# Turning k / F of three sequences with the DMA crossbar instead of TensorE

## The chip, the cores and the metric

The kernel runs on one core of one Trainium2 chip. The metric is the device time of one execution in microseconds (us). TensorE does the matrix products, VectorE (DVE in the rows) and ScalarE (ACT) the elementwise work, GpSimd (POOL) a few small jobs, and SyncE (SP) issues every DMA, all on one hardware queue that 16 DMA engines share.

## What is computed

Gated linear attention over 4 sequences of 768 tokens with 8 heads of 48, then a layer norm with an MLP (384 to 1536 to 384) and a residual, then a Fourier mix over both axes with a second norm, MLP and residual:

```python
for t in range(S):
    state = alpha[:, :, t, :, None] * state + np.einsum('bhd,bhe->bhde', k[:, :, t], v[:, :, t])
    y[:, :, t] = np.einsum('bhd,bhde->bhe', q[:, :, t], state)
...
ch = np.maximum(xn @ w_ch1, 0.0) @ w_ch2        # first MLP, x + ch goes on
...
X = np.fft.fft(np.fft.fft(x, axis=1), axis=2)   # u = x + real(X), then norm, MLP, u + ch
```

Everything is float32.

## The kernel before

The attention is computed in chunks of 128 tokens, all four pairs of heads at once. With F the running product of alpha within a chunk, q is multiplied by F (`q_mul`) and k is divided by it (`k_div`, 112 partitions by 4 x 128 columns). Scores are products of `k_div` and `q_mul`; masked, they are multiplied with v. The state's increment is k transposed times v, so it needs `k_div` with tokens on the partitions: `k_divT`, 128 by 4 x 112. In the kernel before, TensorE turns `k_div` with four transposes into a PSUM bank (`transpose_k`, line 1415), and ScalarE copies the bank to `k_divT` (`copy_kT`, line 780).

Chunks are grouped in units. Sequence 0 is units 0, 1 and 2 (two chunks each); sequences 1 to 3 are units 3 to 8 (three chunks each). The first MLP of unit n runs in 12 slots (j = 0 to 11), and the attention of unit n + 1 is woven into the same slots: this is the order of work on each engine, written out by hand. In a slot TensorE does `pe_up(j)` (9 matmuls of 384 columns into a bank h), `pe_down(j - 2)` (9 matmuls into the accumulators), and then the slot's piece of attention. For the three chunks of a unit these are:

- slots 0, 3, 6: transposes and scores (`scores`, line 1430)
- slots 1, 4, 7: increments (line 1442, waits for `kT_copied`) and the masked product with v (line 1499)
- slots 2, 5, 8: the part that comes from the state (`outputs_carried`, line 1512)

ScalarE does the Relu of slot j (`act_relu`, line 168) and then `side_one`: `copy_kT` in slots 0, 3, 6; `copy_y` (line 794) in 2, 5, 8; two range tests of alpha (`check_above`, `check_below`, line 760) in slots 3 and 4. VectorE does the low half of the split hidden layer (line 173), then masks, state updates (lines 1066 to 1075) and the preparation of coming chunks: `prepare_q` (scan forward, scale q) and `prepare_k` (scan backward, scale k, line 1015), at the slots in `q_slots` and `k_slots`. `k_slots` is `{2: 1, 5: 2}`: chunk 1 in slot 2, chunk 2 in slot 5. Chunk 0 of the next unit is prepared in slot 8 (`next_k_slot`; slot 7 for unit 3, slot 10 for unit 4).

SyncE works through one list. For the unit after the one that is being attended, it loads alpha and q once the range tests are done (`load_qka`, lines 507 to 511), then k, then v (line 517), and then stores the rows of the unit whose MLP is ending (line 521). Twice in the first half of the run it also copies rows of x1 in DRAM into reversed order (`turn_top`, line 540, and `turn_bottom`, line 547); these copies are written with an outer dimension of 3:

```python
def in_thirds(rows):
    return rows.rearrange("r (k c) -> k r c", k=TURN_PARTS)
```

`turn_top(0)` is issued before the loads for unit 7, `turn_bottom(0)` before those for unit 8. The hidden banks h are two, the tiles hT three, so a Relu may be late by about one slot before TensorE waits for it.

Of the kernel before, what the change touches and what calls it, by code (L numbers as in the profile page):

```python
# [7 lines left out]
F32 = mybir.dt.float32  # L8
F32R = mybir.dt.float32r
ALU = mybir.AluOpType  # L10
ACT = mybir.ActivationFunctionType

P = 128
# [33 lines left out]
class Unit:  # L47

    def __init__(self, n, b, c0, size, par):  # L50
        self.n, self.b, self.c0, self.size, self.par = n, b, c0, size, par
        self.base = CHUNKS * b + c0
        self.cols = size * P
        self.scores, self.increments, self.outputs = (0, 3, 6), (1, 4, 7), (2, 5, 8)
        self.q_slots, self.k_slots = {3: 2}, {2: 1, 5: 2}
        self.next_slot, self.next_k_slot, self.next_q_slot = 6, 8, 10
        self.rows_slot, self.range_slot = 9, 3
# [7 lines left out]
    def last(self, c):  # L65
        return self.c0 + c == CHUNKS - 1

    def slot(self, c):
# [15 lines left out]
ONE += [Unit(2 * b + half + 1, b, UT * half, UT, half) for b in range(1, B) for half in range(2)]  # L84
ONE[4].q_slots = {1: 1, 3: 2}
ONE[3].next_k_slot, ONE[3].next_q_slot, ONE[3].rows_slot = 10, None, 8
ONE[-1].k_slots = {2: 1, 4: 2}
N1 = len(ONE)
# [154 lines left out]
def pipeline(nc, qT, kT, aT, v, g_cols, w11, w12, w21, w22, tab_seq, tab_dim, out):  # L243
# [17 lines left out]
    with ExitStack() as ctx:  # L261
# [32 lines left out]
        with ExitStack() as one:  # L294
# [9 lines left out]
            q_mul = sb1("q_mul", [R, UT, PAIRS, P])  # L304
            k_divT = sb1("k_divT", [P, PAIRS, R])
            probs = [sb1(f"probs{i}", [P, PAIRS, P]) for i in range(2)]

# [68 lines left out]
        k_ready = sem("k_ready")  # L376
        kT_summed = sem("kT_summed")
        kT_copied = sem("kT_copied")
        sc_summed = sem("sc_summed")
# [104 lines left out]
        def _(sp):  # L484
# [19 lines left out]

            def load_qka(u):
                chunks = slice(u.c0, u.c0 + UT)
                sp.wait_ge(a_bounded, u.base)
                sp.wait_ge(range_checked, u.n)
                sp.dma_start(a_in[:, :, :], aT[u.b, :, chunks, :]).then_inc(a_loaded, 16)
                sp.wait_ge(q_ready, u.base)  # L510
                sp.dma_start(q_in[:, :, :], qT[u.b, :, chunks, :]).then_inc(q_loaded, 16)
                sp.wait_ge(k_ready, u.base)
                sp.dma_start(k_in[:, :, :], kT[u.b, :, chunks, :]).then_inc(k_loaded, 16)

# [46 lines left out]
            for u in ONE[3:-2]:  # L561
                load_qka(u)
                load_v(u)
                store_x1(u.b - 1, u.c0 // UT)
            for half in range(2):
                sp.wait_ge(stored[half], 16 + 16 * 2)
            turn_top(0, turned[0])
            load_qka(ONE[-2])
            load_v(ONE[-2])
            store_x1(B - 2, 0)  # L570
            turn_bottom(0, turned[0])
            load_qka(ONE[-1])
            load_v(ONE[-1])
            store_x1(B - 2, 1)
            split.dma(sp, TABLES[:PIECES])
            sp.wait_ge(s_ready, ONE_CHUNKS)
            sp.wait_ge(k_ready, ONE_CHUNKS)
# [179 lines left out]
        def _(act):  # L757
# [16 lines left out]
            def check_below(u):  # L774
                act.wait_ge(above_checked, u.n + 1)
                beyond(u, 1).then_inc(range_checked, 1)

            def copy_kT(u, c):
                act.wait_ge(kT_summed, u.base + c + 1)
                act.activation(k_divT[:, :, :], bank[BKU][:, 0:PAIRS * R].rearrange("p (h k) -> p h k", h=PAIRS),  # L780
                               ACT.Copy).then_inc(kT_copied, 1)
# [25 lines left out]

            def side_one(u, slot):
                for c in range(u.size):
                    if slot == u.scores[c]:  # L810
                        copy_kT(u, c)
                    if slot == u.outputs[c]:
                        copy_y(u, c)
                if slot == u.range_slot:
                    check_above(u)
                if slot == u.range_slot + 1:
                    check_below(u)
                for k in TRANSPOSES_ONE.get(slot, ()):
                    high_xT(u, k, g_col[:, k:k + 1])

# [57 lines left out]
            def side_zero(j):  # L879
                if 0 < j < len(ONE_W) - 2:  # L880
                    split.high(act, ONE_W[2 + j])
                side_one(ONE[1], j)

            unit_one(ONE[0], side_zero)
            for u in range(1, N1 - 2):
                unit_one(ONE[u], lambda j: side_one(ONE[u + 1], j))

            for j in range(JH):
                m.act_relu(act, ONE[-2], j)  # L890
                side_one(ONE[-1], j)
                if j == 5:
                    act.wait_ge(s_ready, ONE_CHUNKS)
                    act.wait_ge(k_ready, ONE_CHUNKS)
                if j in (5, 6):
                    split.high(act, TABLES[j - 5])
# [55 lines left out]
        def _(dve):  # L952
# [164 lines left out]
            def side_one(u, following, slot):  # L1117
# [9 lines left out]

                if slot > 1 and u.n != 2:
                    prepare()
# [4 lines left out]
                if slot in u.outputs:  # L1134
                    add_odd(u, u.outputs.index(slot))
                if slot <= 1 or u.n == 2:
                    prepare()
# [268 lines left out]
        def _(pe):  # L1406
# [123 lines left out]
            def side_one(u, slot):  # L1530
                for c in range(u.size):
                    if slot == u.scores[c]:
                        transpose_k(u, c)
                        scores(u, c)
# [220 lines left out]
```

## Time and profile before

| | us |
|---|---|
| median of 3 runs | 770.03 (769.61 to 770.52) |
| profiled execution | 769.62 |
| its span in the trace | 768.1 |
| TensorE busy | 758.4 (99%) |
| VectorE busy | 456.4 (59%) |
| ScalarE busy | 216.2 (28%) |
| GpSimd busy | 56.0 (7%) |

The span is what the trace covers; about 1.5 us of the profiled execution lie around it. The first MLPs with the attention fill about the first 390 us, the second MLPs with the Fourier part the rest. In the timelines below a row is one instruction, or neighbours of one line merged; the first column is its start, the second its length. Matmuls overlap in the array, so what one costs is read from the distance between starts, not from its length.

### The profile page before, as it was taken

What the parts mean: (1) busy time and instruction counts of PE and PEld (TensorE: products, weight loads), DVE (VectorE), ACT (ScalarE), POOL (GpSimd) and SP (SyncE); (2) the same over time, 40 slices, a digit from 0 to 9 for tenths busy, and PEclk for the clock granted to TensorE, in tenths of its full rate; (3) what the DMA queues carried; (4) which work ended last, traced back from release to release, by engine and by line L of the source; (5) the groups of instructions that cost most, each with busy time, mean ns of one, the idle gap of its engine ahead of it and who ended that gap; (6) DMA issues with size and microseconds to landing.
All of it is one profiled execution on the core that took longest, in us unless ns stands there. A gap on an engine that the chain in (4) does not pass through costs nothing.

```text
span 768.1 us, 17057 instructions
## 1 busy us (share of the span) xinstructions
PE 758.4 (99%) x7066; PEld 734.9 (96%) x7066; DVE 456.4 (59%) x1056; ACT 216.2 (28%) x430; POOL 56.0 (7%) x112
## 2 busy tenths in 40 slices
PE   8999999999999999999999999999999999999998
PEld 7889899999999999999999999999999999999998
DVE  7888777756676576675686764347443664342422
ACT  3443232322313223124243332112221223111211
POOL 1100000000000000000005000200021000200000
PEclk9999999999999999999999999999999999999999
DMA  9362223141311413423043421020003000000000
GB/s 243 116 169 74 68 83 90 35 129 43 104 38 65 118 63 100 103 84 135 2 133 128 147 66 52 5 99 32 1 32 103 31 0 31 0 1 32 0 32 32
DMA packets 34956, 54.11 MB, mean 70 GB/s; under 512 B 1932, under 2 KB 29828, under 8 KB 34884
## 3 DMA queue, kind: packets, MB, share of 16 engines
q1 hardware_dynamic: 34884, 53.10, 22.9%
q8 instruction: 52, 0.85, 0.5%
q14 instruction: 20, 0.16, 0.1%
HBM read 43.65 MB, written 13.37 MB: 74 GB/s over the span
## 4 chain that ended last, share of the span: by engine, by line
PE 91%; DVE 5%; issue 3%; ACT 1%; POOL 0%; DMA 0%; POOLq 0%; DVEq 0%; ACTq 0%
PE h L99 14%; PE h L101 12%; PE h L100 12%; PE acc L99 12%; PE acc L101 12%; PE acc L100 12%; PE side_bank L1499 2%; PE side_bank L1521 2%; PE side_bank L100 2%; PE side_bank L101 2%; PE side_bank L1430 2%; PE side_bank L1512 2%; PE side_bank L99 2%; PE side_bank L1442 1%; PE side_bank L1415 1%
## 5 line engine op out<-in xcount | busy, mean ns | idle before, releaser
L173 DVE SCALAR_TENSOR_TENSOR hT_low<-h,hT_high 128x384 fp32r<-128x384 f32 (+1 forms) x204 | 108.2, 531 | 173.4 <-ACT hT_high L168 172.9
L99 PE MATMUL h<-xnT_high,w_high 128*128 128x384 f32 (+1 forms) x612 | 208.1, 340 | 0.9 <-DVE w_low L232 0.9
L168 ACT ACTIVATE hT_high<-h 128x384 fp32r<-128x384 f32 (+1 forms) x204 | 96.4, 473 | 377.0 <-PE h L101 376.8
L101 PE MATMUL h<-xnT_high,w_low 128*128 128x384 f32 (+1 forms) x612 | 199.4, 326 | 0.0
L100 PE MATMUL h<-xnT_low,w_high 128*128 128x384 f32 (+1 forms) x612 | 199.2, 325 | 0.0
L99 PE MATMUL acc<-w_high,hT_high 128*128 128x384 f32 x576 | 194.2, 337 | 1.1 <-DVE hT_low L173 1.1
L101 PE MATMUL acc<-w_high,hT_low 128*128 128x384 f32 x576 | 193.0, 335 | 0.0
L100 PE MATMUL acc<-w_low,hT_high 128*128 128x384 f32 x576 | 192.5, 334 | 0.0
L99 PEld LDWEIGHTS h<-xnT_high,w_high 128*128 128x128 f32 x612 | 115.1, 188 | 5.2 <-DVE w_low L232 1.0
L100 PEld LDWEIGHTS h<-xnT_low,w_high 128*128 128x128 f32 x612 | 115.3, 188 | 0.0
L101 PEld LDWEIGHTS h<-xnT_high,w_low 128*128 128x128 f32 x612 | 115.1, 188 | 0.0
L99 PEld LDWEIGHTS acc<-w_high,hT_high 128*128 128x128 f32 x576 | 108.3, 188 | 1.8 <-DVE hT_low L173 1.7
L100 PEld LDWEIGHTS acc<-w_low,hT_high 128*128 128x128 f32 x576 | 108.4, 188 | 0.0
L101 PEld LDWEIGHTS acc<-w_high,hT_low 128*128 128x128 f32 x576 | 108.1, 188 | 0.0
L992 DVE TENSOR_TENSOR_SCAN F_inv<-a_safe,F_end_inv,zeros 112x127 f32<-112x127 f32 x96 | 38.3, 460 | 0.0
L979 DVE TENSOR_TENSOR_SCAN F<-a_safe,zeros 112x128 f32<-112x128 f32 x96 | 32.8, 404 | 0.3
L640 POOL TENSOR_TENSOR var_eps<-mean_var,eps 128x3 f32<-128x3 f32 (+2 forms) x18 | 5.5, 305 | 355.2 <-DVE mean_var L1082 355.2
L760 ACT ACTIVATE xn_one<-a_in,limits 112x1536 bf16<-112x1536 f32 (+1 forms) x18 | 25.7, 1426 | 5.3 <-DMA a_in<-alpha_dram 5.3
L1499 PE MATMUL side_bank<-v_in,probs 64*64 64x48 f32 x704 | 24.7, 218 | 0.0
L1096 DVE TENSOR_TENSOR xnT_low<-side_bank,xnT_high 128x384 fp32r<-128x384 f32 x24 | 12.5, 554 | 19.8 <-ACT xnT_high L799 19.8
L232 DVE TENSOR_TENSOR w_low<-stage,w_high 128x768 fp32r<-128x768 f32 x24 | 22.6, 949 | 2.4 <-ACT w_high L228 2.2
L1499 PEld LDWEIGHTS side_bank<-v_in,probs 64*64 64x64 f32 x704 | 22.8, 135 | 0.0
(142 smaller groups left out, 757.3 us busy)
## 6 DMA issues: line engine op xcount, KB each, us to landing
stage<-w_dram SPq DMA_DIRECT2D x24, 384.0 KB, 3.4
x_scratch<-x_unit SPq DMA_DIRECT2D x8, 576.0 KB, 3.2
a_in<-alpha_dram SPq DMA_DIRECT2D x6, 672.0 KB, 5.3
q_in<-q_dram SPq DMA_DIRECT2D x6, 672.0 KB, 7.4
k_in<-k_dram SPq DMA_DIRECT2D x6, 672.0 KB, 4.8
v_in<-v_dram SPq DMA_DIRECT2D x6, 576.0 KB, 3.7
xb<-x_scratch SPq DMA_DIRECT2D x4, 576.0 KB, 4.1
xb<-x_turned SPq DMA_DIRECT2D x4, 576.0 KB, 6.9
```

What stands on the lines that cost most here:

```text
L99: pe.matmul(out, wh, xh, start=start, stop=False)
L100: pe.matmul(out, wh, xl, start=False, stop=False)
L101: return pe.matmul(out, wl, xh, start=False, stop=stop)
L168: act.activation(self.hT[0][:, j % H_SLOTS, 0:u.cols], self.hps[j % H_BANKS][:, 0:u.cols], ACT.Relu).then_inc(self.h_high, 1)
L173: dve.scalar_tensor_tensor(out=self.hT[1][:, j % H_SLOTS, 0:u.cols], in0=self.hps[j % H_BANKS][:, 0:u.cols], scalar=0.0, in1=self.hT[0][:, ...
L232: dve.tensor_tensor(self.pieces[n][1][1], self.slot(n), self.pieces[n][1][0], ALU.subtract).then_inc(self.low_done, 1)
L760: return act.activation(excess[:, 0:u.size, :], a_in[:, slots_of(u), :], ACT.Relu, bias=limits[:, i:i + 1], scale=(1.0, -1.0)[i], accum_ou ...
L979: op = dve.tensor_tensor_scan(F[:, s, h, :], a_safe[:, s, h * P:(h + 1) * P], zeros[:, :], 1.0, ALU.mult, ALU.add)
L992: op = dve.tensor_tensor_scan(F_inv[:, s, h, P - 2::-1], a_safe[:, s, first + P - 1:first:-1], zeros[:, 0:P - 1], F_end_inv[:, s, h:h + 1] ...
L1430: op = pe.matmul(score_bank(u, two)[sub, h * SUB:(h + 1) * SUB], k_div[HR[two], s, h, sub], q_mul[HR[two], s, h, sub], start=True, stop=True)
L1499: op = pe.matmul(bank[BSC][sub, cols], probs[head % 2][sub, head // 2, 0:SUB], v_in[sub, s, cols], start=head == 0, stop=False)
L1512: op = pe.matmul(to, q_mul[HR[two], s, h, sub], state[HR[two], (u.state_slot(c), MIDDLE)[i], h, :], start=two == 1 and h == 0, stop=h == P ...
```

## The change

For sequences 1 to 3 (18 of 24 chunks) TensorE no longer turns `k_div`. Instead ScalarE copies it into `k_planes`, taking the 32-bit words apart into two planes of 16-bit halves (`split_k`); SyncE issues one DMA transpose of [112 x 1024] 16-bit elements (`turn_k`, 224 KB), which writes `kT_planes` [128 x 8 x 112]; and ScalarE joins the planes to `k_divT` (`copy_kT`, now from SBUF). Each step waits for the one before; there is one buffer of each.

```diff
-        self.q_slots, self.k_slots = {3: 2}, {2: 1, 5: 2}
+        self.q_slots, self.k_slots, self.split_slots = {3: 2}, {1: 1, 4: 2}, {2: 1, 5: 2}
...
+    def turned_by_dma(self):
+        return self.b > 0
...
-ONE[4].q_slots = {1: 1, 3: 2}
+ONE[4].q_slots = {0: 1, 3: 2}
-ONE[-1].k_slots = {2: 1, 4: 2}
+FIRST_TURNED = CHUNKS
...
+            def turn_k(u, c):
+                if not u.turned_by_dma():
+                    return
+                sp.wait_ge(k_split, u.base + c - FIRST_TURNED + 1)
+                sp.wait_ge(kT_copied, u.base + c)
+                sp.dma_start_transpose(kT_planes[:, :, :], k_planes[:, :]).then_inc(kT_turned, 16)
+
+            def load_unit(u):
+
+                attending = ONE[u.n - 1]
+                turn_k(attending, 1)
+                load_qa(u)
+                turn_k(attending, 2)
+                load_k(u)
+                load_v(u)
+                turn_k(u, 0)
...
             turn_top(0, turned[0])
-            load_qka(ONE[-2])
-            load_v(ONE[-2])
+            load_unit(ONE[-2])
             store_x1(B - 2, 0)
             turn_bottom(0, turned[0])
-            load_qka(ONE[-1])
-            load_v(ONE[-1])
+            load_unit(ONE[-1])
             store_x1(B - 2, 1)
             split.dma(sp, TABLES[:PIECES])
+            turn_k(ONE[-1], 1)
+            turn_k(ONE[-1], 2)
...
+            def split_k(u, c):
+
+                act.wait_ge(k_ready, u.base + c + 1)
+                if u.base + c > FIRST_TURNED:
+                    act.wait_ge(kT_turned, 16 * (u.base + c - FIRST_TURNED))
+                act.activation(k_planes[:, :].rearrange("p (two t) -> p two t", two=2),
+                               flat(k_div[:, u.slot(c), :, :]).bitcast(U16).rearrange("p (t two) -> p two t", two=2),
+                               ACT.Copy).then_inc(k_split, 1)
+
             def copy_kT(u, c):
+                if u.turned_by_dma():
+
+                    act.wait_ge(kT_turned, 16 * (u.base + c - FIRST_TURNED + 1))
+                    act.wait_ge(u_summed, u.base + c)
+                    act.activation(flat(k_divT[:, :, :]).bitcast(U16).rearrange("p (k two) -> p two k", two=2),
+                                   kT_planes[:, :, :].rearrange("p (two h) k -> p two (h k)", two=2),
+                                   ACT.Copy).then_inc(kT_copied, 1)
+                    return
...
+                if slot in u.split_slots and u.turned_by_dma():
+                    split_k(u, u.split_slots[slot])
...
+                if slot == u.next_k_slot + 1 and following and following.turned_by_dma():
+                    split_k(following, 0)
...
-                if slot > 1 and u.n != 2:
+                if slot == 3 and u.n != 2:
                     prepare()
...
-                if slot <= 1 or u.n == 2:
+                if slot != 3 or u.n == 2:
                     prepare()
...
-                        transpose_k(u, c)
+                        if not u.turned_by_dma():
+                            transpose_k(u, c)
```

## Rows read from the trace of the kernel before

**Rows 1.** The page: busy us, share of the span and instructions of each engine.
```profile
PE 758.4 (99%) x7066; PEld 734.9 (96%) x7066; DVE 456.4 (59%) x1056; ACT 216.2 (28%) x430; POOL 56.0 (7%) x112
```

**Rows 2.** Timeline of TensorE: slots 5 and 6 of attending unit 5.
```profile
205.62 0.34 PE L101 MATMUL acc<-w_high,hT_low 128*128 128x384 f32 x1
205.89 0.68 PE L1512 MATMUL side_bank<-state,q_mul 48*64 48x48 f32 x32
...
209.56 0.34 PE L101 MATMUL acc<-w_high,hT_low 128*128 128x384 f32 x1
209.74 0.55 PE L1415 MATMUL side_bank<-ident,k_div 112*128 112x112 f32 x4
210.22 0.69 PE L1430 MATMUL side_bank<-q_mul,k_div 48*64 48x64 f32 x32
```

**Rows 3.** Groups by line and shape: busy us, mean ns, idle time before.
```profile
L228 ACT ACTIVATE w_high<-stage 128x768 fp32r<-128x768 f32 x24 | 20.1, 839 | 4.6 <-DMA stage<-w_dram 2.4 <-PE acc L101 2.1
```

**Rows 4.** Timeline of ScalarE, slots 2 to 4 of attending unit 5.
```profile
193.60 0.49 ACT L794 ACTIVATE x_unit<-side_bank 128x384 f32<-128x384 f32 x1 [1.71 <-PE side_bank L1512]
...
197.72 1.57 ACT L760 ACTIVATE xn_one<-a_in,limits 112x1536 bf16<-112x1536 f32 x1
```

**Rows 5.** Timeline of VectorE, slots 1 and 2 of attending unit 5.
```profile
189.97 0.36 DVE L1075 TENSOR_TENSOR state<-state_sum,F 112x192 f32<-112x192 f32 x1
...
192.40 0.17 DVE L986 RECIPROCAL F_end_inv<-F 112x4 f32<-112x4 f32 x1
...
194.38 0.69 DVE L1015 TENSOR_TENSOR k_div<-k_in,F_inv 112x512 f32<-112x512 f32 x1
```

**Rows 6.** DMA issues by tile: size, and median us from issue to landing.
```profile
x_scratch<-x_unit SPq DMA_DIRECT2D x8, 576.0 KB, 3.2
...
v_in<-v_dram SPq DMA_DIRECT2D x6, 192.0 KB, 7.0
...
out_dram<-u_mirror_out SPq DMA_DIRECT2D x3, 192.0 KB, 1.9
```

**Rows 7.** Timeline of TensorE: increments of unit 3, chunks 1 and 2.
```profile
109.42 0.57 PE L1442 MATMUL side_bank<-v_in,k_divT 64*48 64x48 f32 x32
...
119.44 0.57 PE L1442 MATMUL side_bank<-v_in,k_divT 64*48 64x48 f32 x32
```

**Rows 8.** Timeline of ScalarE: slot 2 of attending unit 3.
```profile
103.91 0.49 ACT L794 ACTIVATE x_unit<-side_bank 128x384 f32<-128x384 f32 x1 [1.31 <-PE side_bank L1512]
```

**Rows 9.** Timeline of the DMA issues (SPq); the length is how long the issue took.
```profile
201.79 0.32 SPq L509 DMA_DIRECT2D a_in<-alpha_dram  x1
...
237.91 5.79 SPq L540 DMA_DIRECT2D x_turned<-x_scratch  x2
...
285.88 8.71 SPq L547 DMA_DIRECT2D x_turned<-x_scratch  x2
300.70 2.86 SPq L509 DMA_DIRECT2D a_in<-alpha_dram  x1
```

**Rows 10.** Windows: busy us of each engine, granted clock, DMA share, GB/s.
```profile
203.00:208.00 5.00, 5.00 (x58) 4.70 (x57) 2.90 (x8) 0.98 (x2) 0.00 (x0) 1.00 0.92 256
208.00:209.00 1.00, 1.00 (x7) 1.00 (x7) 0.47 (x3) 0.49 (x1) 0.00 (x0) 1.00 0.14 37
```

**Rows 11.** The same view around the two reversing copies.
```profile
250.00:252.00 2.00, 2.00 (x68) 1.73 (x66) 0.94 (x3) 1.18 (x2) 0.37 (x1) 1.00 0.22 65
252.00:254.00 2.00, 2.00 (x15) 1.97 (x12) 0.36 (x1) 0.10 (x1) 0.00 (x0) 1.00 0.91 210
...
300.00:304.00 4.00, 4.00 (x79) 3.91 (x79) 1.20 (x4) 1.12 (x3) 0.37 (x1) 1.00 0.22 65
```

**Rows 12.** Timeline of TensorE: increments of chunk 1 in units 5, 6 and 7.
```profile
201.13 0.57 PE L1442 MATMUL side_bank<-v_in,k_divT 64*48 64x48 f32 x32
...
250.59 0.57 PE L1442 MATMUL side_bank<-v_in,k_divT 64*48 64x48 f32 x32
...
300.04 0.57 PE L1442 MATMUL side_bank<-v_in,k_divT 64*48 64x48 f32 x32
```

More of the change, by code:

```diff
@@ L9 @@
 F32R = mybir.dt.float32r
+U16 = mybir.dt.uint16
 ALU = mybir.AluOpType
@@ L305, in pipeline @@
             k_divT = sb1("k_divT", [P, PAIRS, R])
+            k_planes = sb1("k_planes", [R, 2 * PAIRS * P], U16)
+            kT_planes = sb1("kT_planes", [P, 2 * PAIRS, R], U16)
             probs = [sb1(f"probs{i}", [P, PAIRS, P]) for i in range(2)]
@@ L377, in pipeline @@
         kT_summed = sem("kT_summed")
+        k_split = sem("k_split")
+        kT_turned = sem("kT_turned")
         kT_copied = sem("kT_copied")
@@ L503, in load_again, with load_qa @@
                 sp.dma_start(v_in[:, s, :], v[0, :, g, :]).then_inc(first_v[g], 16)
-            def load_qka(u):
+            def load_qa(u):
                 chunks = slice(u.c0, u.c0 + UT)
@@ L511, in load_qka, with load_k @@
                 sp.dma_start(q_in[:, :, :], qT[u.b, :, chunks, :]).then_inc(q_loaded, 16)
+            def load_k(u):
                 sp.wait_ge(k_ready, u.base)
-                sp.dma_start(k_in[:, :, :], kT[u.b, :, chunks, :]).then_inc(k_loaded, 16)
+                sp.dma_start(k_in[:, :, :], kT[u.b, :, u.c0:u.c0 + UT, :]).then_inc(k_loaded, 16)
+            def turn_k(u, c):
[12 more added lines that the diff above has]
+                turn_k(u, 0)
             def load_v(u):
@@ L561, in _ @@
             for u in ONE[3:-2]:
-                load_qka(u)
-                load_v(u)
+                load_unit(u)
                 store_x1(u.b - 1, u.c0 // UT)
@@ L806, in high_first, with side_one @@
                                scale=g_col[:, k:k + 1]).then_inc(xT_high if i else first_high, 1)
-            def side_one(u, slot):
+            def side_one(u, following, slot):
                 for c in range(u.size):
@@ L881, in side_zero @@
                     split.high(act, ONE_W[2 + j])
-                side_one(ONE[1], j)
+                side_one(ONE[1], ONE[2], j)
             unit_one(ONE[0], side_zero)
             for u in range(1, N1 - 2):
-                unit_one(ONE[u], lambda j: side_one(ONE[u + 1], j))
+                unit_one(ONE[u], lambda j: side_one(ONE[u + 1], ONE[u + 2], j))
             for j in range(JH):
                 m.act_relu(act, ONE[-2], j)
-                side_one(ONE[-1], j)
+                side_one(ONE[-1], None, j)
                 if j == 5:
```

## The prediction

> **What bounds the kernel now.** I read the page first. TensorE is busy for 758.4 of 768.1 us, VectorE 456.4, ScalarE 216.2 [rows 1]. So an instruction taken from TensorE is worth its place in TensorE's stream, and work added elsewhere costs nothing until TensorE waits for it. The rest is therefore a question of deadlines, and I read those from the timelines of each engine (who must be done by when), from the list of DMA issues, and from windows of DMA traffic. The kernel repeats itself: units 5, 6 and 7 run with the same spacing (the increments of their chunk 1 start at 201.13, 250.59 and 300.04 [rows 12]), so one unit serves for all, except where the DMA queue holds something else.
>
> **What TensorE gains.** The four transposes stand between the last product of `pe_down` and the scores: that product starts at 209.56, the scores at 210.22, 0.66 us later. Where no transposes stand between, as before the next kind of attention work (205.62 to 205.89), the distance is 0.27 us [rows 2]. So a chunk gives back 0.66 - 0.27 = 0.39 us, and 18 chunks 7.0 us. If the step from products to scores were as short as that from transposes to scores, it would be 0.48 each, 8.6 us.
>
> **What the new chain costs, chunk 1 of an ordinary unit (unit 5).** VectorE: the state update of slot 1 ends at 189.97 + 0.36 = 190.3, the preparation of k lasts from 192.40 to 195.07, 2.7 us [rows 5]; moved behind the state update it is done at 193.0. It delays the low half of slot 2 by about 1 us, which the two spare hidden banks cover. ScalarE: `copy_y` ends at 194.1 [rows 4], so k is ready in time, and the split follows. No row shows a ScalarE copy of 16-bit halves with a stride; the nearest is 128x768 32-bit elements in 839 ns [rows 3], by length 1.1 us for 1024 and 1.0 us for 896 elements. Bounds: half of that (the elements are half as wide) to twice. I take it as it is, since that row is the nearest in kind. Split done at 195.2, DMA issued at 195.3.
>
> The DMA transpose is the large unknown: 224 KB from SBUF to SBUF. The nearest rows are 192 KB from SBUF to DRAM in 1.9 us, 576 KB from SBUF in 3.2 us, and 192 KB that waited behind others in 7.0 us [rows 6]. I call issue to landing X, bound it by 1.9 and 7.0 and take 3.2, the 576 KB row, because the crossbar handles short rows of 16-bit elements and will not be as fast as a plain copy of its size. About 1 us of it is the start (in the windows, loads issued at 201.79 fill the engines from 203 on [rows 9, 10]), so 2.2 us is what remains once its turn has come. The Trainium skill (DMA: Bandwidth & Descriptors, section Latency and other measured facts) states 261 GB/s for a DMA transpose with a non-contiguous middle dimension. By that the 224 KB would move in 0.9 us, and with the page's fixed 2 us the whole would be an estimated 2.9 us; no row here shows a transpose. The sum would be about 1 us better by it.
>
> With X = 3.2 it lands at 198.5, the joining copy ends at 199.5, and the increments want it at 201.13 - 0.39 = 200.7 [rows 12]. It is hidden, with 1.2 us to spare: X may be 4.4. Chunk 2 has the same distances. Its DMA, however, is queued behind the loads of alpha and q. These are issued after the two range tests, which ScalarE now reaches later, since it stands in `copy_kT` until 199.5: each test takes 1.57 us and its accumulator read [rows 4], so with the Relu between them they end near 203.2 and not 201.7. The loads' traffic lasted until about 208.2, 6.4 us after their issue at 201.79 [rows 9, 10]; now until 209.7. Chunk 2's transpose is issued at 208.3, starts at 209.7 and lands at 211.9; copied by 212.9, wanted at about 213.4. Hidden, barely. Chunk 0 of the next unit has over 7 us. In units 4, 5 and 8 I count no loss.
>
> **Unit 3** runs beside an MLP of two chunks, whose slots are shorter. `copy_y` ends at 103.91 + 0.49 = 104.4 [rows 8]; split 105.5, landing 108.7, copy 109.7; increments wanted at 109.42 - 0.39 = 109.0 [rows 7]: 0.7 us lost. Chunk 2: the range tests end at 113.4, the loads' traffic at about 119.4, the transpose lands at 121.6 and is copied at 122.6, wanted at 119.44 + 0.7 - 0.78 = 119.4 [rows 7]: 3.2 us lost. Together 3.9.
>
> **Units 6 and 7** decide. SyncE has issued the reversing copies at 237.91 (`turn_top`) and 285.88 (`turn_bottom`) [rows 9], on the same queue and ahead of `turn_k`. Their traffic runs at 65 GB/s with a share of 0.22, about three and a half engines of 16, until 252 and until 304 [rows 11]: 12 and 16 us of backlog on a few engines. What is issued behind waits: the alpha load of 300.70 took 2.86 us to issue instead of 0.32 [rows 9], and the traffic stayed at 65 GB/s until 304, the other engines doing nothing for it [rows 11]. In the kernel before nobody was in a hurry: the loads come at 251.26 and 300.70. The new transposes of chunk 1 come at 244.8 and 294.7 (rows of unit 5, 49.5 and 98.9 us later), in the middle of the backlog, and their semaphore is full only when the slowest engine is done. So they land at 252 + 2.2 = 254.2 and 304 + 2.2 = 306.2, are copied at 255.2 and 307.2, and are wanted at 250.59 - 0.39 = 250.2 and 300.04 - 0.39 = 299.65 [rows 12]. TensorE stands for 5.0 and 7.5 us. The later range tests push the next loads, and chunk 2 of both loses an estimated 0.5 us each. Queued behind the waiting ScalarE are the range tests and the Relu of slot 4, which TensorE wants only in slot 6, so they add nothing of their own. The Trainium skill (DMA: Bandwidth & Descriptors, section Queues, rings and completion order) says that on each DMA engine descriptors of one issuing queue are consumed in ring order, and that a copy runs on as many engines as its outermost dimensions allow, here 3. The trace agrees with both (share 0.22, blocked issue).
>
> Moving the load of k behind `turn_k` of chunk 2 and the load of the Fourier rows behind the last `turn_k` delays them by a few us; both have over 10 us until VectorE reads them. The added ScalarE work, 18 x (1.1 + 1.0 - 0.5), about 29 us, lies in an engine that is busy 28% [rows 1].
>
> **The sum.** -7.0 (transposes) + 3.9 (unit 3) + 5.0 + 7.5 (units 6 and 7) + 1.0 = +10.4 us. The span goes from 768.1 to 778.5, the profiled execution from 769.6 to 780.0; its median is 0.4 above that, so 780.4. With X = 1.9 unit 3 loses 1.3, the two backlogs 3.7 and 6.2, chunk 2 nothing: +4.2, 774.2. With X = 4.4: unit 3 loses 6.3, the backlogs 6.2 and 8.7, chunk 2 of units 4 to 7 some 1.5 each: +20, 790.
>
> **Rivals.**
>
> Faster, because the backlog doesn't hold the transposes. If the crossbar copy goes by engines or rings that the reversing copies don't use, the 12.5 + 1.0 us fall away. What is left is -7.0 + 3.9 = -3.1, 766.9; with X = 1.9 it is -5.7, 764.3. For it: the share of 0.22 leaves 12 engines free. Against it: the alpha load did not use them. It decides for faster as soon as units 6 and 7 together lose less than 3 us.
>
> Slower by far, because the transpose is slow (X of 6 or more: short rows, much work to issue). Then each chunk 1 and 2 waits in every unit. At X = 6 units 4, 5 and 8 lose 1.6 on each of six chunks, unit 3 9.5, the backlogs 18, chunk 2 of units 6 and 7 3 each: 43 - 7 = +36, 806. Against it: no plain row of this size needs that long unless it queues.
>
> The same mechanism as forecast, and TensorE's clock falls in the two long stalls. Every row of the trace shows a granted clock of 1.00 [rows 10, 11], but none holds an idle TensorE of 5 us. If after each stall it ran at half speed for as long as it had stood, it would lose half of that again, 2.5 + 3.8 = 6.3 us: 786.7. The Trainium skill (TensorE: Matmul & The Clock Gate, Part 1) states that an idle TensorE falls from 2.4 to 1.2 GHz; no run here shows it yet.
>
> No difference (within 0.2%, 1.5 us, which is about what a measurement can tell): the backlog holds only in part, and losses and gain meet.
>
> **How the numbers follow.** Forecast 0.42, clock falling on top of it 0.15, not held 0.22, slow transpose 0.14, no difference 0.07. The likeliest gives 780.4, with its own range 774 to 790. For 8 in 10 I go down to 765, which takes in most of the faster case, and up to 797. Faster by over 0.2% 0.22, within 0.2% 0.07, slower 0.71.
>
> **What would show it.** In the profile after: no L1415 after the first six chunks, and scores 0.27 us behind the last product; the transpose's time from issue to landing near 3 us in units 4, 5 and 8, and no idle TensorE there; idle TensorE of some 5 and 7.5 us ahead of the increments of chunk 1 of units 6 and 7, released by the ScalarE copy, which was itself released by the DMA; a few us ahead of unit 3's chunk 2. The prediction is wrong if the transposes land in the middle of the reversing copies, or if X is above 4.4.

## The result and the profile after

| | before | after |
|---|---|---|
| median, us | 770.06 (769.61 to 770.52) | 789.21 (788.5 to 790.14) |
| profiled execution / its span, us | 769.6 / 768.1 | 790.14 / 788.6 |
| mean granted clock | 1.0 | 0.985 |

The ratio is 1.0249, 95% interval 1.0232 to 1.0267: slower by 19 us. The forecast was 780.4 with a range of 765 to 797. The sign and the places were right, the size was half of what came.

The page of the changed kernel, to be held against [rows 1]: busy time of the engines, the clock in 40 slices, the chain that ended last by engine, and the groups of the joining copy and of the increments (busy us, mean ns | idle time before them and what ended it).

```profile
PE 760.9 (96%) x6994; PEld 735.8 (93%) x6994; DVE 455.6 (58%) x1056; ACT 244.1 (31%) x448; POOL 56.2 (7%) x112
...
PEclk9999998999999999799999999999999999999999
...
PE 85%; DMA 5%; DVE 3%; issue 3%; ACT 2%; SPq 1%; POOL 0%; POOLq 0%; DVEq 0%; ACTq 0%
...
L818 ACT ACTIVATE k_divT<-kT_planes 128x896 uint16<-128x896 uint16 x18 | 22.0, 1222 | 51.9 <-DMA kT_planes<-k_planes 51.9
...
L1489 PE MATMUL side_bank<-v_in,k_divT 64*48 64x48 f32 (+1 forms) x672 | 14.7, 220 | 19.3 <-ACT k_divT L818 19.1
```

TensorE has 72 matmuls fewer (18 x 4) and is nevertheless busy longer, 760.9 against 758.4 us: it ran slower for a while, as the clock row says (8 and 7 in two slices). It stood idle 19.1 us for the joining copy, which itself stood idle 51.9 us for the DMA. Where, the timeline of TensorE says (start, length, instruction; in brackets the idle time before it and who ended it). These are all the waits on the copy:

```profile
110.45 0.57 PE L1489 MATMUL side_bank<-v_in,k_divT 64*48 64x48 f32 x32 [0.46 <-ACT k_divT L818]
...
123.94 0.90 PE L1489 MATMUL side_bank<-v_in,k_divT 64*48 64x48 f32 x32 [3.79 <-ACT k_divT L818]
...
260.19 0.90 PE L1489 MATMUL side_bank<-v_in,k_divT 64*48 64x48 f32 x32 [5.11 <-ACT k_divT L818]
...
319.76 0.89 PE L1489 MATMUL side_bank<-v_in,k_divT 64*48 64x48 f32 x32 [9.70 <-ACT k_divT L818]
```

They are chunks 1 and 2 of unit 3, chunk 1 of unit 6 and chunk 1 of unit 7. The same 32 matmuls last 0.57 us after the first and about 0.90 after the other three: the clock had fallen. Windows over the work behind those three stalls (window, us, busy us of PE, PEld, DVE, ACT, POOL, granted clock, DMA share, GB/s); the clock is back at 1.00 from 130.50, 263.62 and 325.06 on:

```profile
123.94:130.50 6.56, 6.56 (x79) 6.14 (x79) 1.92 (x5) 0.56 (x2) 0.00 (x0) 0.50 0.00 0
...
260.21:263.62 3.41, 3.41 (x67) 3.32 (x68) 1.50 (x5) 3.37 (x5) 0.00 (x0) 0.50 0.02 5
...
319.76:325.06 5.30, 5.30 (x73) 5.21 (x74) 3.31 (x10) 3.40 (x5) 0.36 (x1) 0.50 0.19 24
```

SyncE's issues there, to be held against [rows 9] (the length is how long the issue took):

```profile
113.81 0.32 SPq L517 DMA_DIRECT2D a_in<-alpha_dram  x1
...
117.39 1.22 SPq L530 DMA_TRANSPOSE kT_planes<-k_planes  x1
...
243.09 5.70 SPq L567 DMA_DIRECT2D x_turned<-x_scratch  x2
249.32 7.00 SPq L530 DMA_TRANSPOSE kT_planes<-k_planes  x1
...
296.20 8.96 SPq L574 DMA_DIRECT2D x_turned<-x_scratch  x2
...
305.26 10.58 SPq L530 DMA_TRANSPOSE kT_planes<-k_planes  x1
```

**Where the 20.5 us of the span went.** Each unit begins with ScalarE's first Relu of slot 0; from one to the next is a unit. Timeline of ScalarE, units 3 to 8:

```profile
98.49 0.38 ACT L172 ACTIVATE hT_high<-h 128x256 fp32r<-128x256 f32 x1 [3.12 <-PE h L105]
...
143.37 0.49 ACT L172 ACTIVATE hT_high<-h 128x384 fp32r<-128x384 f32 x1 [2.22 <-PE h L105]
...
191.73 0.49 ACT L172 ACTIVATE hT_high<-h 128x384 fp32r<-128x384 f32 x1 [3.81 <-PE h L105]
...
240.06 0.49 ACT L172 ACTIVATE hT_high<-h 128x384 fp32r<-128x384 f32 x1 [3.81 <-PE h L105]
...
295.05 0.49 ACT L172 ACTIVATE hT_high<-h 128x384 fp32r<-128x384 f32 x1 [3.82 <-PE h L105]
...
355.49 0.49 ACT L172 ACTIVATE hT_high<-h 128x384 fp32r<-128x384 f32 x1 [3.81 <-PE h L105]
```

In the kernel before the same Relus start at 97.23, 135.97, 185.42, 234.88, 284.33 and 333.80; the last three of them:

```profile
234.88 0.49 ACT L168 ACTIVATE hT_high<-h 128x384 fp32r<-128x384 f32 x1 [3.81 <-PE h L101]
...
284.33 0.49 ACT L168 ACTIVATE hT_high<-h 128x384 fp32r<-128x384 f32 x1 [3.81 <-PE h L101]
...
333.80 0.49 ACT L168 ACTIVATE hT_high<-h 128x384 fp32r<-128x384 f32 x1 [3.81 <-PE h L101]
```

Lengths of the units, in us. A clean unit is one without a wait on the copy; unit 3, which is shorter, is held against 38.74 - 1.13.

| | before | after | difference to a clean unit | of it idle | of it clock |
|---|---|---|---|---|---|
| units 4, 5 (clean) | 49.46 | 48.33 | -1.13 against before | 0 | 0 |
| unit 3 | 38.74 | 44.88 | +7.3 | 4.25 | 3.0 |
| unit 6 | 49.46 | 54.99 | +6.7 | 5.1 | 1.6 |
| unit 7 | 49.47 | 60.44 | +12.1 | 9.7 | 2.4 |

The clock's column is what is left after the idle time, 7.0 us in all. The windows above give it a second way: work at half clock loses half its time, and half of 6.56, 3.41 and 5.30 us is 3.3, 1.7 and 2.6, 7.6 in all. So what a stall costs in clock follows from how long TensorE works at half speed behind it, and not from the stall's own length. The gain of six units, 6 x 1.13 = 6.8, against 26.1 of losses makes 19.3; the first 97 us add 1.26 (this execution ran at a clock of 0.83 from 20 to 30 us, before anything of the change had begun). Together 20.5.

### The profile page after: what moved, and what is told of

It reads as the page before. It is cut to its first block, busy times and chain, and to the rows that moved or that the text cites. A ratio compares the mean times of both kernels' runs of the same rounds, so it can differ in the third digit from the quotient of the medians.

```text
span 788.6 us, 16984 instructions
## 1 busy us (share of the span) xinstructions
PE 760.9 (96%) x6994; PEld 735.8 (93%) x6994; DVE 455.6 (58%) x1056; ACT 244.1 (31%) x448; POOL 56.2 (7%) x112
## 4 chain that ended last, share of the span: by engine, by line
PE 85%; DMA 5%; DVE 3%; issue 3%; ACT 2%; SPq 1%; POOL 0%; POOLq 0%; DVEq 0%; ACTq 0%
PE h L103 13%; PE acc L103 11%; PE h L104 11%; PE h L105 11%; PE acc L105 11%; PE acc L104 11%; DMA kT_planes<-k_planes 3%; PE side_bank L1546 2%; PE side_bank L1568 2%; PE side_bank L104 2%; PE side_bank L105 2%; PE side_bank L103 1%; PE side_bank L1489 1%; PE side_bank L1559 1%; PE side_bank L1477 1%
## 5 line engine op out<-in xcount | busy, mean ns | idle before, releaser
L103 PEld LDWEIGHTS h<-xnT_high,w_high 128*128 128x128 f32 x612 | 116.0, 189 | 5.4 <-DVE w_low L236 1.0
L818 ACT ACTIVATE k_divT<-kT_planes 128x896 uint16<-128x896 uint16 x18 | 22.0, 1222 | 51.9 <-DMA kT_planes<-k_planes 51.9
L1489 PEld LDWEIGHTS side_bank<-v_in,k_divT 64*48 64x48 f32 (+1 forms) x672 | 11.6, 130 | 25.3 <-ACT k_divT L818 20.6
L1489 PE MATMUL side_bank<-v_in,k_divT 64*48 64x48 f32 (+1 forms) x672 | 14.7, 220 | 19.3 <-ACT k_divT L818 19.1
L1546 PE MATMUL side_bank<-v_in,probs 64*64 64x48 f32 x704 | 27.2, 230 | 0.0
```

The costliest lines, as they stand in the source:

```text
L103: pe.matmul(out, wh, xh, start=start, stop=False)
L818: act.activation(flat(k_divT[:, :, :]).bitcast(U16).rearrange("p (k two) -> p two k", two=2), kT_planes[:, :, :].rearrange("p (two h) k -> ...
L1489: return pe.matmul(psum[HR[two], h * D:(h + 1) * D], k_divT[rows, h, HR[two]], v_in[rows, c, head * D:(head + 1) * D], start=True, stop=True)
L1546: op = pe.matmul(bank[BSC][sub, cols], probs[head % 2][sub, head // 2, 0:SUB], v_in[sub, s, cols], start=head == 0, stop=False)
```

## The experiments

All kernels start from the changed kernel. A global chunk is 3 (unit - 1) + chunk: 8 is chunk 2 of unit 3, 16 and 19 are chunk 1 of units 6 and 7, 20 is chunk 2 of unit 7. Where TensorE takes a chunk back, the counts that the semaphores are waited for are made per chunk (`dma_before`, `pe_before`), which the diffs leave out.

**Slots alone.** All 24 chunks turned by TensorE; only the preparation of k and q stays in its new slots.

```diff
+BY_PE = set(range(24))
-        return self.b > 0
+        return self.b > 0 and self.base + c not in BY_PE
```

> The changed kernel with every chunk turned by TensorE again: what is left of the change is that k is prepared in slots 1 and 4, unit 4's q in slot 0, and the order of VectorE's work in a slot. Theory (the moved preparation lies in VectorE's idle time): 770.0 within 1 us. Rival (VectorE's low halves come late and TensorE waits): above 772, with idle time of TensorE released by VectorE in units 3 to 8.

Measured: 770.36 (769.67 to 770.85, 10 runs), ratio 0.9995 (0.9982 to 1.0007). The move to slots 1 and 4 costs nothing.

**The two chunks in the backlog back to TensorE.**

```diff
+BY_PE = set(range(6)) | {16, 19}
```

> The changed kernel, but chunk 1 of units 6 and 7 is turned by TensorE as before; the other 16 chunks stay with the DMA. Theory (their transposes wait behind the reversing copies, nothing else in these units is wrong): the two stalls of 5.1 and 9.7 us go, with them the 1.5 and 2.3 us that TensorE lost at half clock behind them, and two chunks of transposes come back (0.8 us): 789.2 - 18.6 + 0.8 = about 771.4. Chunk 2 of both units may now lose up to 1 us, since its spare time is gone. Rival (the transposes are slow wherever they are hurried): the stalls move to chunk 2 of the same units, and the time stays above 780.

Measured: 771.40 (770.81 to 773.09, 10 runs), ratio 1.0014 (1.0001 to 1.0027), clock 0.996. Two chunks of 18 carry 17.8 of the 19 us. The waits left are 0.47 and 3.87 us in unit 3 and 0.72 in chunk 2 of unit 7.

**Three chunks back.** Unit 3's late chunk as well.

```diff
+BY_PE = set(range(6)) | {8, 16, 19}
```

> As the run with two chunks back on TensorE, and chunk 2 of unit 3 as well (the other 15 chunks stay with the DMA). Theory: unit 3's stall of 3.9 us and the 3.0 us lost at half clock behind it go, one chunk of transposes comes back (0.4): 771.4 - 6.5 = 764.9, faster than the kernel before by 5 us; what is left idle is 0.5 us in unit 3's chunk 1 and 0.7 in unit 7's chunk 2. Rival (the time between was hidden elsewhere, the gain per chunk is less than 0.39 us): not below 768.

Measured: 766.34 (765.62 to 767.96, 4 runs), ratio 0.9951 (0.9934 to 0.9968), clock 0.998. The third chunk gave 5.1 us of the 6.5 expected, more than its stall of 3.87 us. In the kernel with two chunks back TensorE works from 122.85 to 128.08 at a granted clock of 0.50 behind that stall, which is gone here. In this trace the clock was at half from 21.39 to 24.80 instead, ahead of anything that the change touches. With 15 chunks on the DMA the kernel is 3.8 us faster than before; 0.46 and 1.03 us of waits are left.

**A lighter backlog.** The reversing copies in 12 parts and not 3, everything else as in the changed kernel.

```diff
-TURN_PARTS = 3
+TURN_PARTS = 12
```

> The changed kernel, but the reversing copies are written in 12 parts of 128 bytes a row instead of 3 of 512 bytes, so they use 12 engines. If their time goes by bytes for each engine, the backlog shrinks to a quarter (12 and 16 us to 3 and 4), the transposes of units 6 and 7 land about 3 us after issue, and the stalls with their clock cost go: 789.2 - 18.6 = 770.6. If it goes by rows (each engine has the same number), the backlog stays as long and now lies on 12 engines: the time stays at 789 or rises. Either way the landing of both transposes follows the end of the copies' traffic.

Measured: 770.93 (769.47 to 772.25, 10 runs), ratio 1.0006 (0.9996 to 1.0015). The whole loss in units 6 and 7 goes although no transpose was moved. Windows of this kernel during the two reversing copies (window, us, busy us of PE, PEld, DVE, ACT, POOL, granted clock, DMA share, GB/s), and its issues:

```profile
246.00:248.00 2.00, 2.00 (x19) 1.98 (x12) 0.36 (x1) 1.54 (x3) 0.00 (x0) 1.00 1.20 130
...
292.00:294.00 2.00, 2.00 (x13) 1.89 (x11) 1.90 (x5) 0.49 (x1) 0.00 (x0) 1.00 1.22 133
```
```profile
247.62 1.28 SPq L530 DMA_TRANSPOSE kT_planes<-k_planes  x1
...
296.35 3.46 SPq L530 DMA_TRANSPOSE kT_planes<-k_planes  x1
```

**The DMA's own queue.** ScalarE issues the transposes itself, right behind its split, so that they share no queue with the reversing copies.

```diff
-                sp.wait_ge(k_split, u.base + c - FIRST_TURNED + 1)
-                sp.wait_ge(kT_copied, u.base + c)
-                sp.dma_start_transpose(kT_planes[:, :, :], k_planes[:, :]).then_inc(kT_turned, 16)
+                return
...
+                act.wait_ge(k_split, u.base + c - FIRST_TURNED + 1)
+                act.wait_ge(kT_copied, u.base + c)
+                act.dma_start_transpose(kT_planes[:, :, :], k_planes[:, :]).then_inc(kT_turned, 16)
```

> The changed kernel, but ScalarE issues the DMA transposes itself, behind its split, so that they come on its own hardware queue; loads and reversing copies stay on SyncE's. Theory A (what holds them is the order of one queue): they land some 3 us after issue also in units 6 and 7, and chunk 2 of unit 3 no longer waits behind the loads; stalls of 14.8 us and 3.8 us of lost clock go, of unit 3's 7.3 us at least 4: 789.2 - 22.6 = about 766, perhaps 1 or 2 us more for the 1.2 us that each issue holds ScalarE. Theory B (the few DMA engines are busy, whatever the queue): the transposes still land when the reversing copies are over, and the time stays within 3 us of 789.

Measured: 795.36 (791.5 to 803.2, 4 runs), ratio 1.0349 (1.0273 to 1.0425). Neither number came. Timeline of TensorE and ScalarE of this kernel:

```profile
126.04 0.89 PE L1490 MATMUL side_bank<-v_in,k_divT 64*48 64x48 f32 x32 [5.71 <-ACT k_divT L819]
263.05 0.57 PE L1490 MATMUL side_bank<-v_in,k_divT 64*48 64x48 f32 x32 [2.57 <-ACT k_divT L819]
315.55 0.57 PE L1490 MATMUL side_bank<-v_in,k_divT 64*48 64x48 f32 x32 [0.95 <-ACT k_divT L819]
332.44 0.57 PE L1490 MATMUL side_bank<-v_in,k_divT 64*48 64x48 f32 x32 [4.17 <-ACT k_divT L819]
```
```profile
116.69 1.24 ACTq L812 DMA_TRANSPOSE kT_planes<-k_planes  x1
124.79 1.20 ACT L819 ACTIVATE k_divT<-kT_planes 128x896 uint16<-128x896 uint16 x1 [6.38 <-DMA kT_planes<-k_planes]
```

The backlog lost its hold: chunk 1 of unit 6 waits 2.57 and not 5.11 us, that of unit 7 0.95 and not 9.70, and no issue of a transpose takes over 2.2 us. The reversing copies' last packets end at 263.50 and 322.08, the transposes land at 261.78 and 314.27, before them. But chunk 2 came later in every unit, in unit 3 8.1 us after its issue (116.69 to 124.79) against 5.3. What had changed there is that the loads were no longer behind it: SyncE issued the load of k at 115.60, 1.1 us ahead of the transpose, on another queue. That is a suspicion until the load is taken away.

**The loads held back.** As the kernel before this one, but SyncE issues the loads of k and v only after chunk 2's transpose has landed; and in a second kernel those of alpha and q too, for which it also calls `turn_k(attending, 2)` ahead of `load_qa(u)`.

```diff
-                return
+                if u.turned_by_dma() and c == 2:
+                    sp.wait_ge(kT_turned, 16 * (u.base + c - FIRST_TURNED + 1))
```

> ScalarE issues the transposes from its own queue, as in the run before of that kind, but SyncE issues the loads of k and v only after chunk 2's transpose has landed, so that of the loads only alpha and q are in flight beside it. Theory S (the late chunk 2 comes from sharing the 16 engines with the loads): the landing of chunk 2, 5.2 to 8.4 us without the hold, falls to 4 to 6 us, since alpha and q, issued about 3 us ahead of it, are done about 4 us after its issue; unit 3's stall of 5.71 us falls to some 3, unit 7's of 4.17 to some 2, and the kernel from 795 to about 788. Theory Q (a transpose on ScalarE's queue is slow by itself when another queue is active at all, or a landing there is seen late): chunk 2 stays at 5.2 to 8.4, and the time at 795 or above.

> As the kernel with the hold, but SyncE holds back all four loads, alpha and q too, until chunk 2's transpose has landed: nothing else is in flight beside it. Theory S: chunk 2 lands 2.9 to 3.3 us after its issue in every unit, as on an idle machine; unit 3's stall falls to about 1 us (5.71 less 8.1 - 3.0), the stalls of chunk 1 of units 6 and 7 (2.57, 0.95) stay. Against the first theory would be a landing of chunk 2 above 4 us. The time then depends on whether the loads, some 6 us later, are still in time for VectorE: about 780 if they are, with new waits of VectorE on alpha or q if they are not.

Measured: 778.43 (776.31 to 780.55, 4 runs), ratio 1.0098 (1.0079 to 1.0116) with k and v held; 792.95 (789.92 to 796.47), ratio 1.0311 (1.0276 to 1.0345) with all four. The chunk 2 transposes land, from issue to the start of the copy, in units 3 to 8:

| us | 3 | 4 | 5 | 6 | 7 | 8 |
|---|---|---|---|---|---|---|
| own queue | 8.1 | 5.2 | 6.7 | 6.0 | 8.4 | 6.7 |
| k, v held | 5.6 | 4.1 | 4.2 | 3.8 | 3.0 | 2.9 |
| all four held | 4.6 | 3.0 | 3.0 | 3.5 | 3.0 | 2.9 |

So a transpose on ScalarE's queue is not slow by itself, and the chunk 2 transposes were late because they shared the engines with the loads; holding two of them gave 17 us, to 778 where 788 was expected. One landing speaks against that alone: with all four loads held, unit 3's took 4.6 us, and above 4 us had been named as a sign against the theory. No load ran beside it, but one instruction packet of 16 KB did (queue, kind, packets, MB, share of the engines between 116.0 and 121.5):

```profile
q10 hardware_dynamic: 928, 0.23, 22.8%
q8 instruction: 1, 0.02, 1.1%
```

That packet held its engine for 0.94 us, in the middle of the transpose's packets. Over all traces kept here the 88 transposes beside which nothing else ran landed 2.89 to 2.95 us after their issue, and the 29 beside which only instruction packets ran 2.91 to 4.55 us. No kernel here moves these packets, so their part is read from the traces and not tested.

ScalarE of the kernel with k and v held in unit 3, and VectorE of the one with all four held:

```profile
116.61 1.24 ACTq L811 DMA_TRANSPOSE kT_planes<-k_planes  x1
122.24 1.20 ACT L818 ACTIVATE k_divT<-kT_planes 128x896 uint16<-128x896 uint16 x1 [3.91 <-DMA kT_planes<-k_planes]
```
```profile
125.81 0.96 DVE L1017 TENSOR_SCALAR a_safe<-a_in 112x1536 f32<-112x1536 f32 x1 [6.30 <-issue]
```

The second shows where the time of the other went: VectorE stood 6.30 us ahead of its first read of alpha in unit 3 (that load was issued at 121.23 and landed 4.5 us later), 26.7 us in five units, and TensorE waited behind it, 13.1 us in five waits on the state. I had expected about 780 and given the loads of alpha and q room that they do not have. Chunk 1 of units 6 and 7 still landed 7.1 and 7.4 us after its issue with k and v held (7.0 and 5.4 without the hold), and TensorE waited 2.59 and 2.88 us: the own queue weakens the backlog, but does not remove it.

**The clock.** To learn what the halved clock costs, TensorE works instead of standing: 128x128 matmuls of the identity, ahead of the increments of chunks 8, 16 and 19, into a bank that is overwritten; a wait for `u_read` ahead of the scores lets the bank be read first. First 30, 42 and 80 of them, then half.

```diff
+                for _ in range({8: 15, 16: 21, 19: 40}.get(g, 0)):
+                    pe.matmul(bank[BKU][:, 0:P], ident[:, :], ident[:, :], start=True, stop=True)
...
+                        elif u.base + c in {8, 16, 19}:
+                            pe.wait_ge(u_read, u.base + c)
```

> The changed kernel with small matmuls on the identity put into TensorE's stream ahead of the three increments that wait long: 30 in unit 3 (chunk 2), 42 in unit 6 and 80 in unit 7 (chunk 1), 0.11 us each, so that they end before the wait does. The stalls stay. Theory (behind each stall TensorE ran at half clock, which cost 3.0, 1.5 and 2.3 us): the granted clock stays at 1.00 and the time falls by 6.8 to about 782.4. Rival (these microseconds are something else, such as late Relus): no change, 789.

> As the run with matmuls on the identity ahead of the three long waits, with half as many: there each took 0.23 us and not 0.11, so that they outlasted the waits. Now 15, 21 and 40 (3.4, 4.8 and 9.1 us) ahead of waits of 3.8, 5.1 and 9.7 us. The stalls stay, the granted clock stays at 1.00: 789.2 - 6.8 = 782.4. If the microseconds behind the stalls aren't the clock: 789.

Measured: 798.03 (797.46 to 798.74), ratio 1.0353 (1.0318 to 1.0388), clock 1.0 for the first; 785.59 (783.99 to 786.46), ratio 1.0192 (1.0175 to 1.0209), clock 0.999 for the second. TensorE in the first:

```profile
118.86 6.86 PE L1533 MATMUL side_bank<-ident 128*128 128x128 f32 x60
311.63 18.03 PE L1533 MATMUL side_bank<-ident 128*128 128x128 f32 x160
```

Each 32-bit matmul is two in the trace and takes 0.23 us, twice what I had counted, so the filling lasted 34.4 us where 18.6 us of stalls were to be filled: +15.8, and the time rose by only 8.8. The missing 7.0 are the clock, which stayed at full. That agrees with the table above (3.0 + 1.6 + 2.4 = 7.0). In the second kernel only 3.6 us came back, since a filling just as long as the stall let other waits through (2.24 us ahead of chunk 2 of unit 7, 1.82 left ahead of chunk 1): 17.4 us of filling and 5.8 us of waits stand for 18.6 us of stalls, 4.6 more, and with 7.0 of clock that makes 2.4 of the 3.6. The Trainium skill (TensorE: Matmul & The Clock Gate, Part 1) states that an idle TensorE falls from 2.4 to 1.2 GHz; the traces agree, with a granted clock of 0.50 behind the three long stalls and of 1.00 in the same places with the filling.

**Unit 3's chunk 2 first.** Its transpose is issued ahead of the loads of alpha and q.

```diff
+                if attending.n == 3:
+                    turn_k(attending, 2)
+                    load_qa(u)
```

> The changed kernel, but in unit 3's turn SyncE issues the transpose of chunk 2 before the loads of alpha and q for unit 5, not behind them. Theory A (of the 5.3 us from issue to landing 2.4 are the loads in front, the rest is that the slots are short): it lands 2.9 us after issue, the stall of 3.8 us shrinks to 1.4, the clock doesn't fall behind so short a stall: 789.2 - 5.4 = 783.8. Theory B (the short slots alone): 789 as before, landing unchanged at 5.3. The loads of unit 5 come some 4 us later, which costs nothing.

Measured: 787.92 (786.25 to 789.79, 4 runs), ratio 1.0231 (1.0209 to 1.0253): 1.3 us gained of the 5.4 expected. The transpose landed after 3.8 us and not 5.3, but TensorE still waited, and the clock still fell, for 3.4 us. The loads, which came later, cost something after all: at 127.77 TensorE waits 0.92 us for VectorE's state. And behind chunk 1 of unit 6, whose stall is the same (5.08 us), TensorE worked 4.5 us at half clock in this execution and 3.4 in that of the changed kernel, so the price of a stall varies by more than half a us. Timeline and a window of TensorE:

```profile
121.54 0.72 PE L1493 MATMUL side_bank<-v_in,k_divT 64*48 64x48 f32 x32 [2.38 <-ACT k_divT L822]
```
```profile
122.00:124.00 2.00, 2.00 (x47) 1.91 (x39) 0.47 (x1) 0.00 (x0) 0.00 (x0) 0.50 1.01 295
```

So queueing behind the loads is 1.4 us of unit 3's lateness. The rest is that a transpose alone, with its copy, is too long for a unit with short slots: in the changed kernel it is issued at 117.39 and wanted at 120.15, 2.8 us later, and the two take 2.9 and 1.2 us at best.

**The best of both.** Twelve parts, and chunk 8 back on TensorE; then chunks 7, 8 and 20.

```diff
-TURN_PARTS = 3
+TURN_PARTS = 12
+BY_PE = set(range(6)) | {8}
```

> The changed kernel with both repairs: reversing copies in 12 parts, and chunk 2 of unit 3 turned by TensorE (17 of 18 chunks by the DMA). Theory (causes add up): 770.9 of the run with 12 parts, less the 3.9 us stall and 3.0 us of half clock in unit 3, plus 0.4: 764.4. Rival (the repairs share a part of their gain, as when a stall in unit 3 gave others time): above 766.

> As the run before it, with chunk 1 of unit 3 and chunk 2 of unit 7 on TensorE as well, where 0.47 and 0.73 us of idle TensorE were left against 0.39 us for a chunk of transposes: 764.4 - 1.2 + 0.8 = 764.0, no difference that can be measured. If it is faster by 1 us or more, those waits cost more than their length.

Measured: 765.17 (764.27 to 765.72, 5 runs), ratio 0.9934 (0.9921 to 0.9948), clock 1.0; and 765.51 (764.7 to 766.45), ratio 0.9939 (0.9925 to 0.9953). The first beats both kernels: 4.9 us faster than before. The page says the same as its time:

```profile
PE 752.9 (99%) x6998; PEld 727.9 (95%) x6998; DVE 455.3 (60%) x1056; ACT 242.6 (32%) x447; POOL 55.9 (7%) x112
```

TensorE is busy 5.5 us less than in [rows 1] and again 99% of the span; 17 x 0.38 = 6.5 us are gained and 1.8 us of waits left. The second made no difference; its expectation named the wrong chunk, since with 12 parts the wait of 0.73 us is that of unit 7's chunk 1 and not its chunk 2.

## Why the prediction was half right

**The gain of 7.0 us** was right. The scores follow the last product of `pe_down` by 0.26 us (215.12 to 215.38), as [rows 2] has it where no transposes stand between, and a clean unit is 1.13 us shorter, 0.38 us a chunk.

**X = 3.2** was close, a little too long. With nothing in its way a transpose lands 2.9 us after its issue; 12 of the 18 lie between 2.9 and 3.7, the others behind or beside loads or in the backlog. The row of 576 KB in [rows 6] was the right neighbour, and the Trainium skill's figure (DMA: Bandwidth & Descriptors, Latency and other measured facts), from which an estimate of 2.9 us had come, agrees with it still better. The split took 1.05 us (1.1 forecast), the join 1.22 us (1.0). Units 4, 5 and 8 have no wait, as predicted: [rows 7, 12] as deadlines were read rightly.

**Unit 3, 3.9 us** by the sum: 0.46 and 3.79 us of idle time, 4.25 in all. The size of each wait was right (0.7 and 3.2 forecast). What failed is the step that this stall leaves the clock alone; it cost 3.0 us more.

**Unit 6, 5.0 us**: 5.11. **Unit 7, 7.5 us**: 9.70. The mechanism was the one forecast; the end of the backlog, what follows it, the join and the moment of the wish were each a little off. The issue of unit 7's transpose ended at 315.84 (305.26 + 10.58), and it landed at 318.48, 23.4 us after the unit's start and not 21.9. The step that failed is the reading of [rows 11]. There the traffic rises at 252 and 304, and the prediction took that for the end of the reversing copies. It is only the moment at which other transfers begin on the other engines: the copies' own 512-byte packets go on at the same pace, to 252.42 and 306.22 in the kernel before and to 257.64 and 317.21 in the changed one. For unit 7 that end came 22.2 us after the unit's start where 19.7 had been put, 2.5 too early; the transpose then landed 1.3 us behind the last such packet, and not 2.2. Together 1.6 of the 2.2 us that were missing; 0.2 are the longer join, and 0.3 that the increments wanted their operand 15.0 us after the unit's start (310.06) and not 15.3, since chunk 0's transposes, gone too, also lay ahead of them. In unit 6 the end was put 0.5 us too early and the remainder 0.9 us too long, and with the join and the earlier wish this cancels: that 5.0 came so near to 5.11 is partly luck. Windows of the changed kernel over this stall, and the traffic from 300 to 319 in 40 slices:

```profile
310.00:314.00 4.00, 0.07 (x1) 0.00 (x0) 0.00 (x0) 0.00 (x0) 0.00 (x0) 1.00 0.22 65
314.00:315.00 1.00, 0.00 (x0) 0.00 (x0) 0.00 (x0) 0.00 (x0) 0.00 (x0) 0.91 0.21 65
315.00:318.00 3.00, 0.00 (x0) 0.00 (x0) 0.00 (x0) 0.00 (x0) 0.00 (x0) 0.50 1.08 117
...
324.00:325.00 1.00, 1.00 (x4) 1.00 (x4) 1.00 (x3) 0.00 (x0) 0.00 (x0) 0.50 0.93 104
325.00:326.00 1.00, 1.00 (x7) 1.00 (x7) 0.79 (x3) 0.49 (x1) 0.00 (x0) 0.97 0.88 313
```
```profile
DMA  2222223222222222222222222222222299226500
GB/s 65 66 65 67 65 65 100 65 67 65 65 65 66 67 65 65 70 59 66 65 67 65 65 66 65 67 65 65 65 66 65 68 201 163 66 59 107 116 0 0
```

Three and a half engines' worth of traffic at 65 GB/s, every compute engine idle; then two slices in which the other engines move their part of the transpose; then the copy's rest alone at 66 and 59; and only then the part of the transpose that lay behind it. The Trainium skill (DMA: Bandwidth & Descriptors, Queues, rings and completion order) has descriptors of one issuing queue consumed in ring order on each engine; the landings agree, and that the same transposes land in 7.0 and 5.4 us from a queue of their own agrees too.

**Chunk 2 of units 6 and 7, 1.0 us**: nothing, no wait in either. The stall of chunk 1 delays the wish for chunk 2 as much as its making.

**The clock, 0 us in the sum**: 7.0 us. This is the largest error, and it was a choice: I had it as a rival at a chance of 0.15 and 6.3 us, with the argument that no row of the trace holds an idle TensorE of 5 us. Rows that cannot show a thing are no evidence against it. The rival's size was near in sum by luck, since its rule of half the stall gives 9.3 us for the three stalls (18.6 us), and it was wrong in its places: it fell in unit 3 too, where it had not been counted, and cost less than half the stall in units 6 and 7.

Forecast sum +10.4; measured +19.1 by the medians. The clock is 7.0 of the difference, unit 7's wait 2.2, unit 3 and unit 6 0.5, and against them the 1.0 of chunk 2.

**The rivals.** "Backlog does not hold" fell: the transposes waited for it to the end, and the two chunks that met it cost 17.8 us. "Slow transpose" fell with a landing of 2.9 us. The clock on top of the forecast is what came.

**Open.** Why a packet of 128 bytes takes 16.7 ns where one of 512 takes 27.0, which keeps 12 parts from being four times as fast as 3; and why a queue of its own shortens the landing behind the backlog only to 5.4 to 7.4 us.

## What to carry to other kernels

A transfer that was nobody's hurry may sit behind a copy of few parts for 16 us at no cost; before a transfer with a deadline is put on the same queue, list what the queue holds at each of its issues, and either spread that copy over the engines or leave those few instances on the old path. The change was worth its place in 15 of 18 chunks as it stood, and in 17 with the copies in 12 parts; the other three decided its sign. A stall of TensorE of a few us can cost more than itself, so it is to be counted with the clock behind it.

## What the runs showed of the hardware

- The DMA transpose of 224 KB of 16-bit elements from SBUF to SBUF: issue 1.22 us on SyncE, 1.24 on ScalarE, landing 2.89 to 2.95 us after the issue in all 88 cases with nothing beside it, 928 packets each (16,704 in 18). A 16 KB packet of instructions beside it, about 1 us long, makes it 2.91 to 4.55. ScalarE's copies that take 32-bit words apart into planes and join them: 1.05 us for 112x1024 and 1.22 us for 128x896 elements of 16 bits, 1.03 and 1.36 ns an element of a partition. The first reads with a stride and the second writes with one; no run separates that from their shapes.
- The issue of a DMA behind a long copy on the same queue can itself take long: 7.00 and 10.58 us for the transposes in the backlog, against 1.22. Everything behind it in SyncE's list waits too.
- A copy from DRAM to DRAM in 3 parts of 512-byte packets moves 65 GB/s at a share of 0.22, in 12 parts of 128-byte packets about 130 GB/s at a share of 1.20; the packets take 27.0 and 16.7 ns.
- Packets of another queue make a transpose longer. In units 3 to 7 chunk 2 landed in 5.2 to 8.4 us beside the loads of alpha, q and k, in 3.0 to 5.6 beside those of alpha and q, in 3.0 to 4.6 beside none of them.
- The granted clock was at half (1.2 GHz) behind stalls of 2.38, 3.79, 5.11 and 9.70 us, at 1.00 behind those of 0.46 and 0.95, and came back 3.4 to 6.6 us after the work had begun again. It need not fall at once: with the own queue the 32 matmuls behind the stalls of 2.57 and 4.17 us still took 0.57 us, and the clock fell to 0.50 only 1.7 and 0.6 us after the work had begun. In the traces kept here every stall of 2.38 us or more had half clock in its course or within 1.8 us behind it, and none of the five from 2.07 to 2.25 us had. A stall is not needed, though: in four executions the clock was at half from 21 to 25 us, with no idle time of TensorE above 0.4 us in the 18 us before. Of the stall of 9.70 us the clock's share was 2.4 us, of that of 3.79 us 3.0: it does not grow with the stall.
